# GpSimd's scatters of the first routed layer, sent four together behind an expert's last gather and otherwise one tile later

## What is computed

```python
y = irfft(rfft(x, 2*S) * rfft(h, 2*S))[:, :S]      # long convolution, batch 4, S = 5696

# layer 1: 8 experts with exactly N/8 = 2848 rows each
order = argsort(-(x @ w_gate).flatten())           # best (row, expert) pairs first
# a row goes to the first expert in this order that still has room
out[mask] = relu(x[mask] @ w1[e]) @ w2[e]          # w1: 128x1024, w2: 1024x128

# layer 2: each row to the expert of its largest logit, weighted by its softmax
out[mask] = gate_w[mask] * (relu(x[mask] @ w1[e]) @ w2[e])
```

## Time and profile before

| what | value |
|---|---|
| time, median of 3 runs | 2356.96 us (2347.2 to 2360.69) |
| the profiled execution, its own time | 2342.93 us |
| its span in the trace | 2341.1 us |
| TensorE busy | 1975.6 us (84%) |
| VectorE busy | 1284.0 us (55%) |
| ScalarE busy | 947.6 us (40%) |
| GpSimd busy | 726.8 us (31%) |
| mean granted TensorE clock | 0.917 of 2.4 GHz |

### The profile page before, as it was taken

The page is one execution under the profiler, slowest core; times in us unless marked ns, Lnnn a source line. Parts: engine busy times, 40 slices in busy tenths (PEclk is TensorE's granted clock), DMA queues, the critical chain, the costliest instruction groups (busy, mean ns, idle before and its releaser), DMA issues.

```text
span 2341.1 us, 36407 instructions
## 1 busy us (share of the span) xinstructions
PE 1975.6 (84%) x10729; PEld 1530.3 (65%) x10729; DVE 1284.0 (55%) x4137; ACT 947.6 (40%) x2046; POOL 726.8 (31%) x618
## 2 busy tenths in 40 slices
PE   7886999799634978788887888796959999999998
PEld 3343444355423857566666667584759999999998
DVE  2224777422378756656574756511246666666665
ACT  3334887422111423333332323252425555555554
POOL 0001000000144244352516263446423443434434
PEclk9898999899855999898988989797979999999999
DMA  7776999778783011111101111101168888888885
GB/s 194 258 245 215 312 310 308 200 208 206 212 299 123 19 34 28 36 33 31 35 27 38 33 31 39 45 25 39 32 211 289 276 279 283 276 287 278 280 282 176
DMA packets 161018, 382.35 MB, mean 163 GB/s; under 512 B 29813, under 2 KB 88876, under 8 KB 135581
## 3 DMA queue, kind: packets, MB, share of 16 engines
q1 hardware_dynamic: 120749, 287.59, 39.0%
q10 hardware_dynamic: 11696, 57.94, 7.1%
q0 software_dynamic: 28480, 35.66, 5.4%
HBM read 273.07 MB, written 109.13 MB: 163 GB/s over the span
## 4 chain that ended last, share of the span: by engine, by line
PE 63%; DVE 11%; DMA 9%; issue 8%; another core or an unknown queue 4%; SPq 2%; POOL 2%; ACT 1%; ACTq 0%; DVEq 0%; POOLq 0%
PE bank L842 9%; PE bank L928 8%; PE bank L929 8%; PE bank L930 8%; DMA arena<-in_dft_mid_dram 4%; PE bank L772 3%; PE bank L863 3%; PE bank L751 3%; PE bank L865 3%; PE bank L752 2%; PE bank L864 2%; DMA arena<-in_h_dram 2%; PE bank L672 2%; DVE ge L1371 2%
## 5 line engine op out<-in xcount | busy, mean ns | idle before, releaser
L1131 ACT ACTIVATE arena<-bank 128x356 f32<-128x356 f32 x512 | 237.9, 469 | 557.1 <-PE bank L865 437.7
L842 PE MATMUL bank<-arena 128*128 128x356 f32 x1024 | 416.9, 491 | 1.0 <-issue 0.9
L1528 DVE SCALAR_TENSOR_TENSOR hlo<-bank,hhi 128x374 fp32r<-128x374 f32 x544 | 297.8, 548 | 191.1 <-ACT hhi L1164 138.8
L1657 POOL DMA_INDIRECT out_dram<-orow,slot x204 | 247.0, 1211 | 381.0 <-DVE slot L1567 327.0
L1164 ACT ACTIVATE hhi<-bank 128x374 fp32r<-128x374 f32 x544 | 262.9, 483 | 250.8 <-PE bank L930 211.1
L863 PE MATMUL bank<-xhi,wsp 128*128 128x356 f32 x512 | 281.5, 550 | 18.8 <-issue 9.4
L1634 POOL DMA_INDIRECT sorted<-arena,slot x192 | 205.4, 1070 | 180.3 <-DVE slot L1309 115.2
L1625 POOL DMA_INDIRECT xr<-conv_y,idx x192 | 209.4, 1091 | 153.4 <-PE bank L811 83.8
L928 PE MATMUL bank<-xhi,wsp 128*128 128x374 f32 x544 | 193.1, 355 | 3.6 <-DMA wsp<-w_split 3.6
L842 PEld LDWEIGHTS bank<-arena 128*128 128x128 f32 x1024 | 192.6, 201 | 2.2 <-issue 1.5
L1606 POOL TENSOR_TENSOR wsp<-arena,wsp 128x1024 fp32r<-128x1024 f32 x16 | 41.8, 2614 | 468.5 <-ACT wsp L1081 468.5
(11 more groups left out here) (216 smaller groups left out, 3669.6 us busy)
## 6 DMA issues: line engine op xcount, KB each, us to landing
wsp<-w_split SPq DMA_DIRECT2D x136, 1024.0 KB, 5.4
arena<-spec_a SPq DMA_DIRECT2D x90, 320.0 KB, 3.4
spec_a<-arena ACTq DMA_DIRECT2D x16, 1600.0 KB
spec_b<-arena SPq DMA_DIRECT2D x90, 256.0 KB, 3.6
arena<-spec_b SPq DMA_DIRECT2D x16, 1280.0 KB
arena<-in_dft_mid_dram SPq DMA_DIRECT2D x90, 192.0 KB, 4.3
arena<-in_moe_w_dram SPq DMA_DIRECT2D x32, 512.0 KB, 5.5
w_split<-wsp ACTq DMA_DIRECT2D x16, 1024.0 KB, 6.4
```

The source lines that it names most:

```text
L842: r = mm(bank[Z1[t % 2]][:, 0:T1], w2raw[u][:, f * D:(f + 1) * D], h32[:, f, :], start=(f == 0), stop=(f == FC - 1))
L1131: nc.scalar.activation(h32[:, f, :], bank[H1[q % len(H1)]][:, 0:T1], ACT.Relu).then_inc(m_hh[0], 1)
L1528: v.scalar_tensor_tensor(hl[:, f, 0:T], bank[f % 4][:, 0:T], 0.0, hh.bitcast(F32)[:, f, 0:T], ALU.max, ALU.subtract).then_inc(m_hl[m_], 1)
L1657: nc.gpsimd.indirect_dma_start(out=out[:, :], out_offset=place(slot2[u][0:n, s:s + 1]), in_=orow[3 * u + s][0:n, :], in_offset=None, bound ...
```

## The change

Only the rule `after` is another. For the tiles before tile 51 a scatter was issued 8 tiles behind its own. Now it is 9 tiles, if the tile's place in its batch group (`r = (t + 1) % 8`) is 4 or more; that is tiles 3 to 6 of each expert. The four tiles 7, 8, 9 and 10 (and so on every 8 tiles) are all issued behind the same gather, that of tile 15: an expert's last. The first three scatters, of tiles 0 to 2, go behind the gather of tile 7.

```diff
-            after = lambda t: t + (8 if t < PER_E * (E - 2) + 3 else 5)
+            def after(t):
+                if t >= PER_E * (E - 2) + 3:
+                    return t + 5
+                r = (t + 1) % PER_E
+                return t + 9 if r >= GB else t + 8 - r
+
             sends = 0
             for t in range(NT1):
                 if t % PER_E == 0:
```

## The result

The changed kernel takes 2341.84 us (median of 17 runs, 2329.76 to 2348.59). The kernel before, run beside it, takes 2356.96 us (17 runs, 2346.73 to 2364.24). The ratio is 0.9942 [0.9928, 0.9956] (the bracket is the 95% interval): 13.7 us less, where 67 were forecast. The sign was right and the size was not.

What follows compares the result with a forecast made beforehand. TensorE was taken as the bound, its signals late during long unbroken runs of GpSimd's indirect DMAs. Terms -7.8 - 56.8 + 18.6 - 6.6 - 4.6 - 9.8 = -67.0 us took 2356.96 to 2290.0 us, range 2258 to 2352.

Steps and rivals of the forecast that it cites:

- The second gather earlier: First to second transpose, experts 1 to 5: without a scatter ahead, spacing becomes expert 0's 6.54 us; 7.8 us less.
- The next three tiles: Second to fifth tile, experts 1 to 5: without scatters the lateness goes, 2.3 us of honest work stays; 56.8 us less.
- Scatters one tile later: Fifth tile's gather goes ahead of the scatter waiting for target rows; no cost and no gain counted.
- the theory: TensorE's signals arrive late when GpSimd issues indirect DMAs without a break for some 20 to 27 us.
- The four together: Scatters behind an expert's last gather: one late hand-over of 3.72 us charged per expert, five experts; 18.6 us more.
- Rows 6: Trace rows of expert 0: twelve gathers unbroken for 19.3 us without loss, taken as a run length that does no harm.
- The cover of `w1_low`: Idle time of the next expert's `w1_low` behind the four scatters: 18.2 us left; if gone, each us more delays that expert.
- Experts 6 and 7: Late hand-over at expert 6 goes (6.6 us less); expert 7's tile 56 gains 4.6, its next two tiles 9.8.
- C: Rival, chance 0.10: the four scatters bring the lateness with them, so the kernel is slower, +15 us, 2372 us.
- B: Rival, chance 0.15: lateness belongs to an expert's start, only the gather's wait goes; -12.4 us, 2344.6 us.
- A: Rival, chance 0.20: part of the lateness stays, half the gain at the next three tiles comes; -28.8 us, 2328 us.

Runs made afterwards that it cites:

- second_gather_only: Kernel before, with only the first scatter behind an expert's first gather moved behind its second gather, at experts 1 to 6; ratio to before 0.9995.
- together_only: Half of the change on the kernel before: tiles 7 to 10 sent together behind an expert's last gather, tiles 3 to 6 still 8 behind; ratio 0.9938.
- later_only: Half of the change on the kernel before: tiles 3 to 6 of each eight sent one tile later, the other four still 8 behind; ratio 0.9979.
- paced_again: Changed kernel; in the run of four, each tile's scatters wait until those of the tile before have landed; 2276.19 us, ratio to before 0.9727.
- paced_all: paced_again plus waits for landed gathers at an expert's third and fourth gathers and before expert 7's scatters; 2257.23 us, ratio to before 0.9654.
- spread_again: Changed kernel; in the run of four, each tile's scatters are held until a later step of TensorE; 2276.27 us, ratio to before 0.9739.
- gathers_twice: Changed kernel plus a second, unread set of three gathers at each of the first four tiles of experts 0 to 5; 2397.2 us, ratio to before 1.0253.

## Why the prediction was off, by its own steps

1. *The second gather earlier*, forecast -7.8, measured -14.3 on A and -14.2 on C in its own window. The new spacing is 5.2 us, not expert 0's 6.54; expert 0 was the wrong model, for its window has VectorE's listing in it. But what the window gained isn't what the kernel gained: on chip B 8.9 of 14.2 us come back before the fifth tile, and second_gather_only keeps 1.8 on C. So terms 1 and 2 can only be judged together.

2. *The next three tiles*, forecast -56.8, measured -33.1 on A and -36.0 on C. With term 1 that is -47.4 and -50.2, where -64.6 was forecast. From first tile to fifth the forecast comes to 43.6 us per expert; chip B, where nothing is late, takes 43.5 in together_only, so the floor of both terms together was right. What was wrong is that all the lateness would go: 47.0 us remained on A and 45.2 on C, 3.5 and 1.7 above that floor. Right mechanism, over-sized. No run on A or C tells how much of this gain is due to the scatters that left and how much to the fifth tile's gather, which now goes ahead of the wait for target rows.

3. *Scatters one tile later*, forecast 0. On chip B 0 (178.05 us from fifth to eighth in later_only). On A +8.1 and on C +7.4, not forecast. The traces show where. Before, the scatters behind an expert's last gather had to wait for target rows (at expert 2 until 1063.56), so only three DMAs stood in a row there. Now the scatters of the tile before come first. Their rows are ready, and six DMAs follow one another just while VectorE waits for a digit's counts. Changed kernel at expert 2, timelines of POOL, PE and DVE:

```profile
1042.20 1.02 POOL L1625 DMA_INDIRECT xr<-conv_y,idx  x1 [3.46 <-PE bank L811]
...
1048.70 0.98 POOL L1634 DMA_INDIRECT sorted<-arena,slot  x1 [0.30 <-issue]
```
```profile
1046.24 1.42 PE L772 MATMUL bank<-ge,expt 128*128 128x128 bf16 x24
...
1049.35 0.29 DVE L1382 TENSOR_TENSOR dcnt<-bank,tabs 128x128 f32<-128x128 f32 x1 [2.68 <-remote]
```

The same digit before (timelines of POOL, PE and DVE):

```profile
1051.97 0.99 POOL L1625 DMA_INDIRECT xr<-conv_y,idx  x1 [0.30 <-issue]
...
1053.43 1.42 PE L772 MATMUL bank<-ge,expt 128*128 128x128 bf16 x24
...
1054.30 0.29 DVE L1382 TENSOR_TENSOR dcnt<-bank,tabs 128x128 f32<-128x128 f32 x1 [0.47 <-PE bank L772]
```

In the changed kernel this read waits for 2.4 to 2.7 us at all of experts 1 to 5 on A and on C, and sixth to seventh transposes take 13.0 us, not 11.4. The variants with pauses elsewhere keep it (182.5 to 188.5 from fifth to eighth). In paced_again, paced_all and spread_again there are four experts where the third gather took 1.9 us and not 1.0; at these the read is on time (after 0.58 us at expert 3 of paced_again), and the stretch takes 11.4. That fits the theory, but nothing was changed to bring it about.

4. *The four together*, forecast +18.6, measured +38.9 on A and +36.9 on C, and another 15 us at tile 54 (24.69 us, undisturbed 9.72). **This is the step that failed.** I charged one late hand-over of 3.72 us per expert at five experts, on the ground that 15.6 us of run are shorter than the 19.3 us that did no harm at expert 0. The run cost 5 to 7.5 us at each of six experts, and not 3.7; expert 0's end (38.80 us for 32.85, by nine DMAs, 11.3 us) and expert 6 were not in the sum at all. Rows 6 were read wrongly: 11.9 of the 19.3 us of expert 0's run lie ahead of its second tile's transposes, where TensorE is busy for 1.89 of 6.54 us and hands over little. A run that did no harm there is no bound elsewhere. Even six DMAs cost 1.5 us at the place of point 3, while at an expert's end, between pauses, they cost nothing. The cover of `w1_low` was never the matter.

5. *Experts 6 and 7*, forecast -21.0, measured -0.7 on A and -3.0 on C. The hand-over at expert 6's start went (22.42 us for its first two tiles, now 13.91), and the wait for ScalarE at tile 56 went too, but tile 54's 15 us took it back. The transposes of expert 7 (timeline of PE, changed kernel, against the earlier trace rows):

```profile
1589.43 0.53 PE L811 MATMUL bank<-tabs,xr 128*128 128x128 f32 x3 [1.66 <-DMA xr<-conv_y,idx]
...
1597.15 0.85 PE L811 MATMUL bank<-tabs,xr 128*128 128x128 f32 x3 [3.92 <-DMA xr<-conv_y,idx]
```

The first now waits for its rows instead, and the second more so, because tile 57's gather stands behind three scatters (now of tile 51, before of tile 48). Tile 57 takes 23.83 us (25.91 before); on C paced_all takes it from 22.65 to 11.69, so 11 of them were lateness.

On the rivals. *C* named the mechanism that decided: lateness comes with the four. It got a chance of 0.10 and the condition that 85% of the run's length is lost; 6.5 of 15.6 us were. *B*'s number, 2344.6, is nearest to the measured 2341.8, but on A and C it comes from a difference of large terms. Only on chip B is it about what happens: the gather's wait gives 5.3 us and the wait for ScalarE 4.6, of the 12.5 us that lie between later_only and together_only. That both kinds of chip show 0.6% is chance. *A* is true of term 2 alone. The rule that I cited against the change, VectorE shutting GpSimd out of its descriptor rings (the Trainium skill, "DMA: Bandwidth & Descriptors", section "SWDGE vs HWDGE vs iDMA"), did not decide: at expert 2 the twelve scatters of the run took 0.97 to 1.00 us each, also beside VectorE's operations.

What is shown: on chips A and C, signals of TensorE reach ScalarE and VectorE late during a run of indirect DMAs without a pause; more DMAs make it worse, fills don't, and pauses of 1.7 to 2.1 us in the issuing, one after every three DMAs, cure it at an expert's end. What stays open is why, and why chip B has none of it. A pile of unfinished transfers looks unlikely, by the view of DMA activity from 1055 to 1085 us in the changed kernel (40 slices of 0.75 us, busy share in tenths, then GB/s):

```profile
DMA  0000001202025599994202021100000000000000
GB/s 0 0 0 0 0 34 56 85 22 69 7 90 44 208 317 355 347 320 144 64 13 90 0 90 40 31 0 0 0 0 0 0 0 0 0 0 0 0 0 0
```

The last slice with traffic is 1073.75 to 1074.5, directly behind GpSimd's last scatter (1073.06). The block in the middle is the load of the next weights; it stands in the paced run too. Whether the rate of issue or the number in a row decides isn't told apart: both change with a pause. No single number in a row does decide: what a run costs depends on what TensorE hands over beside it.

## What to carry to other kernels

When an engine's long run of DMAs makes others late, moving the run moves the loss. Break it: three pauses of some 2 us in a run of twelve, or one of 4 to 5 us, turned a gain of 0.6% into one of 2.2 to 2.7%, and pauses in every long run made it 3.5%. In the order of before, without slack for them, pauses only moved the run. A run counts by all that stands in it, so look also at where a moved instruction joins two short runs. Price every place where the moved work will stand, by what the others hand over there, also at the first and the last round of the loop.

## What was not expected of the hardware

- The same kernel takes 2258 us on one chip, 2339 on another, and 2357 where the result was measured, with a granted clock of 0.921 to 0.927 in the runs on the first and of 0.912 to 0.921 in those on the second. With pauses in every long run chip C reaches 2257.23 us and 0.930 in its profiled execution. The first layer, from its first transpose to its last, then takes 848.9 us there, for 928.6 before; the variants on chip B take 835.0 to 847.5. Before itself has no profile on chip B, but by these numbers most of the difference between the chips was this lateness.
- In the rows shown the lateness hardly outlasts the run. At expert 2 of the changed kernel ScalarE's Relu starts 4.4 us after the end of its matmul and 0.7 us after that of GpSimd's last scatter (1073.06). In gathers_twice VectorE's last late read (775.11) starts 2.3 us after GpSimd's run.
